# Order of the feed-forward products and of the Fourier steps changed, and U's remainders at a change of batch formed on Pool instead of VectorE

## The reference, cut to what matters

```python
# q, k, v: (2, 8, 768, 64); x below is (2, 768, 512); FF = 2048
x = local_and_global_attention(q, k, v)          # 96 local keys, 8 global ones
h = x.transpose(0, 2, 1) @ U @ V                 # rank 32, mixes the sequence
u = x + h.transpose(0, 2, 1)
x = u + relu(u @ w_ch1) @ w_ch2                  # layer 1, per batch
mixed = real(fft(fft(x, axis=1), axis=2))
u = x + mixed
un = (u - mean(u)) / sqrt(var(u) + 1e-6)
out = u + relu(un @ moe2_w_ch1) @ moe2_w_ch2     # layer 2, per batch
```

## Time and profile before

| what | value |
|---|---|
| median of 3 runs | 742.73 us (742.34 to 746.5) |
| profiled execution: its own time | 743.1 us |
| profiled execution: span of the core | 741.3 us |
| TensorE busy, share of the span | 682.5 us, 92% |
| VectorE / ScalarE / Pool busy | 421.2 / 308.4 / 377.6 us |

### The profile page before, as it was taken

How to read it: one execution, slowest core, us unless ns; L and a number is a source line. 1 busy time by engine, 2 the same in 40 slices (tenths; PEclk the granted TensorE clock), 3 DMA queues, 4 the chain that set the end, 5 groups by cost and what they waited for, 6 DMA issues and landing times.

```text
span 741.3 us, 10239 instructions
## 1 busy us (share of the span) xinstructions
PE 682.5 (92%) x3672; PEld 605.1 (82%) x3672; DVE 421.2 (57%) x903; ACT 308.4 (42%) x665; POOL 377.6 (51%) x365
## 2 busy tenths in 40 slices
PE   8949989999999988799997979999897889999997
PEld 6949889888898877688886869787786778899886
DVE  7526665544445386764675466653865485454544
ACT  4636676442433353234332444332343364334430
POOL 0140143244355899553453796555444876665621
PEclk9988999999999989999999999999999999999999
DMA  8332224012112313111110111111111022121132
GB/s 240 132 124 97 98 97 143 15 55 79 38 56 81 108 58 93 57 43 43 58 57 29 58 57 57 57 57 57 31 56 56 30 70 73 62 81 57 57 114 86
DMA packets 50532, 54.07 MB, mean 73 GB/s; under 512 B 4432, under 2 KB 37328, under 8 KB 50352
## 3 DMA queue, kind: packets, MB, share of 16 engines
q1 hardware_dynamic: 50480, 53.40, 22.9%
HBM read 53.39 MB, written 3.15 MB: 76 GB/s over the span
## 4 chain that ended last, share of the span: by engine, by line
PE 67%; DVE 12%; POOL 8%; ACT 6%; issue 5%; DMA 1%; DVEq 0%; SPq 0%; POOLq 0%; ACTq 0%
PE yP L753 10%; PE yP L755 9%; PE yP L754 9%; PE Yb L732 3%; PE Yb L733 3%; PE Yb L734 3%; PE aP L647 3%; PE aP L621 3%; PE Zb L732 2%; PE Zb L734 2%; PE Zb L733 2%; DVE Y L1249 2%; PE Xb L732 2%; PE Xb L733 2%; PE Xb L734 2%
## 5 line engine op out<-in xcount | busy, mean ns | idle before, releaser
L518 POOL TENSOR_TENSOR WCL<-w_stage,WCH 128x512 fp32r<-128x512 f32 (+1 forms) x128 | 154.7, 1230 | 204.9 <-ACT WCH L952 204.9
L1249 DVE TENSOR_TENSOR Y<-yP,Y 128x512 f32<-128x512 f32 x192 | 129.7, 684 | 89.4 <-PE yP L755 89.1
L753 PE MATMUL yP<-WOH,hidH 128*128 128x512 f32 x384 | 155.6, 405 | 24.6 <-DVE Y L1249 22.8
L755 PE MATMUL yP<-WOH,hidL 128*128 128x512 f32 x384 | 153.1, 399 | 0.0
L754 PE MATMUL yP<-WOL,hidH 128*128 128x512 f32 x384 | 152.6, 397 | 0.0
L524 POOL TENSOR_TENSOR WOL<-o_stage,WOH 128x512 fp32r<-128x512 f32 x64 | 86.0, 1366 | 46.6 <-ACT WOH L959 46.6
L753 PEld LDWEIGHTS yP<-WOH,hidH 128*128 128x128 f32 x384 | 73.5, 191 | 43.7 <-DVE Y L1249 28.2
L962 ACT ACTIVATE hidH<-Xb 128x384 fp32r<-128x384 f32 x64 | 31.4, 491 | 182.1 <-PE yP L755 174.3
L1242 DVE SCALAR_TENSOR_TENSOR hidL<-Xb,hidH 128x384 fp32r<-128x384 f32 x64 | 35.6, 556 | 89.8 <-ACT hidH L962 89.8
L755 PEld LDWEIGHTS yP<-WOH,hidL 128*128 128x128 f32 x384 | 73.0, 190 | 16.2
L754 PEld LDWEIGHTS yP<-WOL,hidH 128*128 128x128 f32 x384 | 73.3, 191 | 11.0
(11 more groups left out here) (216 smaller groups left out, 1360.3 us busy)
## 6 DMA issues: line engine op xcount, KB each, us to landing
w_stage<-w_in SPq DMA_DIRECT2D x128, 128.0 KB, 2.3
o_stage<-w_out SPq DMA_DIRECT2D x32, 512.0 KB, 3.3
V<-v_win SPq DMA_DIRECT2D x8, 704.0 KB, 7.0
K<-k_win SPq DMA_DIRECT2D x8, 644.0 KB, 5.4
Q<-q_t SPq DMA_DIRECT2D x16, 192.0 KB, 3.4
Y<-x_scratch SPq DMA_DIRECT2D x8, 384.0 KB
out<-Y SPq DMA_DIRECT2D x12, 256.0 KB, 3.7
CSraw<-seq_dft SPq DMA_DIRECT2D x1, 1348.0 KB, 7.3
```

Source lines behind the costliest of these rows:

```text
L518: nc.gpsimd.tensor_tensor(WCL[:, g % 2, u0:u1, :, :], w_stage[:, 1 + u0:1 + u1, :, :], hi32(WCH[:, g % 2, u0:u1, :, :]), ALU.subtract).the ...
L753: nc.tensor.matmul(bank[:, :], hh, WOH[:, h % 2, f, :], start=f == 0, stop=False)
L755: mm = nc.tensor.matmul(bank[:, :], hl, WOH[:, h % 2, f, :], start=False, stop=f == 1)
L1249: nc.vector.tensor_tensor(y, yP[t % 2][:, :], y, ALU.add).then_inc(s_yadd, 1)
```

## The change

- `ITEMS` becomes P1 P6 L0 P5 L1 P2 L2 L3 P7 L4 L5 P4 P3: P5 and P6 change places, and P3 and P4. The relu and `lo` of (f 1, half 1) move from P7 (ScalarE) and L4 (VectorE) to L5. The first output tiles wait for three of the round's four remainders, and only L3 for all four.
- `FFN_SLOT` is 35; the last `first_split` is at slot 33.
- The Fourier steps stand only in gaps 1 to 8 of a round (`CALM`), one position per gap, and `combine` is cut into `combine` and `stats`.
- ScalarE's UCH of a sum waits for that sum alone, of a RAW slice for none, and stands in other gaps.
- UCL at a change is formed by Pool in two instructions per factor, in its own order: four factors ahead of the change's round, P7's before `w_lo`, P4's and P3's behind it.
- Pool does `u_sums` ahead of `w_sums(g+2)`, and `u_sums(0, k)` ahead of `w_sums(1)`.
- CSH is made in three instructions, CSL in six, CDL in two.

```diff
-ITEMS = ("P1", "P5", "L0", "P6", "L1", "P2", "L2", "L3", "P7", "L4", "L5", "P3", "P4")
+ITEMS = ("P1", "P6", "L0", "P5", "L1", "P2", "L2", "L3", "P7", "L4", "L5", "P4", "P3")
+CALM = (1, 2, 3, 4, 5, 6, 7, 8)
...
-        FFN_SLOT = 33
+        FFN_SLOT = 35
...
-            for product, late in zip(PRODUCTS, (2, 4, 6, 7, 10, 13, 15)):
+            for product, late in zip(PRODUCTS, (3, 5, 7, 8, GAPS + 2, GAPS + 4, GAPS + 6)):
                 put(GAPS * (g - 1) + late, "split", c, product)
...
+            def at(n, *what):
+                put(GAPS * (first + n // len(CALM)) + CALM[n % len(CALM)], "fourier", b, *what)
+            for n, *what in ((0, "fold", 0, 0), (1, "fold", 0, 1), (2, "fold", 0, 2), (3, "split", 0), (4, "edge"), (6, "seq", 0, 0),
+                             (7, "fold", 1, 0), (8, "seq", 0, 1), (8, "fold", 1, 1), (9, "fold", 1, 2), (10, "split", 1),
+                             (12, "seq", 1, 0), (13, "seq", 1, 1), (15, "seq", 2, 0), (16, "mid")):
+                at(n, *what)
+            for n in range(18, 42):
+                for i in range(HT):
+                    for late, *what in ((0, "dim", i, 0), (1, "dim", i, 1), (2, "combine", i, 0), (3, "stats", i, 0), (4, "combine", i, 1),
+                                        (5, "stats", i, 1), (6, "norm", i, 0), (7, "norm", i, 1), (7, "turn", i, 0), (8, "turn", i, 1)):
+                        if n == 18 + 7 * i + late:
+                            at(n, *what)
...
+            def split(c, name):
+                j, op = PRODUCTS.index(name), FACTORS[name][1]
+                pool.wait_ge(s_uch, splits(c) + j + 1)
+                for k in range(KF):
+                    nc.gpsimd.tensor_tensor(UCL[:, op, k, :], factor(op)[:, k, :], hi32(UCH[:, op, k, :]), ALU.subtract).then_inc(s_ucl, 1)
             w_sums(0)
             w_lo(0)
-            w_sums(1)
             for k in range(KD):
                 u_sums(0, k)
+            w_sums(1)
             for g in range(ROUNDS):
+                if g in CHANGES:
+                    split(CHANGES.index(g), PRODUCTS[4])
                 if g + 1 < ROUNDS:
                     w_lo(g + 1)
+                if g in CHANGES:
+                    for name in PRODUCTS[5:]:
+                        split(CHANGES.index(g), name)
                 o_lo(g)
-                if g + 2 < ROUNDS:
-                    w_sums(g + 2)
+                if g + 1 in CHANGES:
+                    for name in PRODUCTS[:4]:
+                        split(CHANGES.index(g + 1), name)
                 if g + 2 in CHANGES:
                     for k in range(KD):
                         u_sums(CHANGES.index(g + 2) + 1, k)
+                if g + 2 < ROUNDS:
+                    w_sums(g + 2)
                 if g == FPAIRS - 1:
...
-                if j == 0:
-                    act.wait_ge(s_tadd, 2 * KD * (c + 2))
+                if op >= T1:
+                    act.wait_ge(s_tadd, 2 * KD * (c + 1) + {T1: 2, T2: 6, T4: 7, T3: 8}[op])
...
-                if t == 0:
-                    pe.wait_ge(s_hidl, 4 * (h + 1))
+                if t % HT == 0:
+                    pe.wait_ge(s_hidl, 4 * h + (3 if t == 0 else 4))
```

More of the change, by code:

```diff
@@ L373, in fourier_slots @@
         def fourier_slots(b):
[L374 to L390, removed]
+            first = FPAIRS * (b + 1) + 1
+            def at(n, *what):
[10 more added lines that the diff above has]
+                            at(n, *what)
         for b in range(B):
@@ L566, in _ @@
                     nc.gpsimd.tensor_copy(FIX[:, :], CSraw[:, HT * (CN + HALF):SEQ_COLS]).then_inc(s_csh, 1)
-                    nc.gpsimd.tensor_copy(CSH[:, :, :], CSdft).then_inc(s_csh, 1)
-                    pool.wait_ge(s_csh, 2)
-                    nc.gpsimd.tensor_tensor(CSL[:, :, :], CSdft, hi32(CSH[:, :, :]), ALU.subtract).then_inc(s_csplit, 1)
+                    for t in range(HT):
+                        nc.gpsimd.tensor_copy(CSH[:, t, :], CSdft[:, t, :]).then_inc(s_csh, 1)
+                    pool.wait_ge(s_csh, 1 + HT)
+                    for t in range(HT):
+                        for c in (slice(0, CN), slice(CN, CN + HALF)):
+                            nc.gpsimd.tensor_tensor(CSL[:, t, c], CSdft[:, t, c], hi32(CSH[:, t, c]), ALU.subtract).then_inc(s_csplit, 1)
                 if g == FPAIRS:
@@ L573, in _ @@
                     nc.gpsimd.tensor_copy(CDH[:, :, :], CDraw).then_inc(s_csh, 1)
-                    pool.wait_ge(s_csh, 4)
-                    nc.gpsimd.tensor_tensor(CDL[:, :, :], CDraw, hi32(CDH[:, :, :]), ALU.subtract).then_inc(s_csplit, 1)
+                    pool.wait_ge(s_csh, HT + 3)
+                    for k in range(KF):
+                        nc.gpsimd.tensor_tensor(CDL[:, k, :], CDraw[:, k, :], hi32(CDH[:, k, :]), ALU.subtract).then_inc(s_csplit, 1)
         @block.tensor
@@ L983, in item_done @@
                     relu(0, 0, Xb)
-                elif item == "P7":
+                elif item == "L5":
                     act.wait_ge(s_x22, g + 1)
@@ L1357, in fourier @@
                     nc.vector.tensor_tensor(y[:, DS + 1:D], y[:, DS + 1:D], right[:, DS - 1:0:-1], ALU.add).then_inc(s_u2, 1)
+                elif what == "stats":
+                    i, part = at
+                    n = HT * b + i
+                    y = Y[:, base + HT * part + i, :]
                     dve.wait_ge(s_u2, 2 * (2 * n + part) + 2)
@@ L1382, in fill @@
                         mix(*what)
-                    elif kind == "split":
-                        split(*what)
                     elif kind == "fourier":
```

38 lines of the change are left out of this document (20 added, 18 removed).

## The result

The change made the kernel slower. The median went from 742.81 us (five runs) to 765.81 us (five runs, 764.39 to 770.62), a ratio of 1.0307 with a 95% interval of 1.0275 to 1.0339. The forecast was 728.2 us, with a range of 717 to 739. The profiled execution took 770.62 us, its span is 768.6; it is the slowest of the five, 4.8 us above their median.

A forecast was written before the change was run, and what follows sets the result against it. The prediction took TensorE as the bound, so its waits count. Terms -8.9 + 4.5 + 1.6 - 6.2 - 4.5 - 1.0 = -14.5 took the profiled 743.1 us to 728.6, 728.2 as a median, range 717 to 739.

The forecast's parts named there:

- Part 1: Start, near 50 us: u_sums(0, k) ahead of w_sums(1) shrinks TensorE's 9.48 us wait to 2.4, without slow clock; -8.9 us.
- Part 2: Changes of batch: Pool forms U's remainders, its queue delaying P7, P4 and P3; +4.5 us at the first, +1.6 later.
- Part 3: Rounds 10 to 14 and 18 to 22: Fourier steps in the calm gaps remove TensorE's waits; -6.2 and -4.5 us.
- (b): Rival: Pool becomes the bound and runs slower than its rows, its stretches half longer; 796 us, chance 0.06.
- Part 4: Last round: L0 waits for the third remainder, not the fourth, while P3 runs; -1.0 us.
- (a): Rival: only the start gains; the calm gaps trade waits for others, so part 3's terms are 0; 738.9 us, chance 0.15.
- (c): Rival: later pairs' loads or a clock still at 0.5 hold the start, leaving 3 of 8.9 us; 734.1 us, chance 0.10.

The follow-up runs named there:

- e4: The kernel before, with only u_sums(0, k) put ahead of w_sums(1) on Pool: 735.88 us, ratio 0.9902.
- c1: The changed kernel with the Fourier steps back in the old gaps and U's remainders back on VectorE: 720.49 us, ratio 0.9682 against the kernel before.
- e1: The changed kernel with only its Fourier steps put back into the old gaps, over all 13: 735.39 us, ratio 0.9896 against the kernel before.
- e7: The changed kernel with Pool forming only a small part of W's remainders in rounds 9 to 13 and 17 to 21, the rest left out: 744.34 us.
- e5: The changed kernel with its own order of Fourier steps spread over all 13 gaps, 1.6 items apart: 738.53 us, ratio 0.9908 against the kernel before.
- e6: The changed kernel, calm gaps kept, with the turns and the second block's seq steps one gap later: 748.84 us, ratio 1.0066 against the kernel before.
- c2: c1 with all Fourier steps of batch 0 four gaps later: 722.08 us, ratio 0.9703 against the kernel before.
- c3: c1 with only the Fourier steps of the first eight slots of batch 0 four gaps later: 718.70 us, ratio 0.9657 against the kernel before.
- e3: The changed kernel with U's remainders at a change formed by VectorE again: 749.66 us, ratio 1.0098 against the kernel before.
- e9: e1 with the tables CSH and CSL formed behind o_lo(8), one round later: 742.61 us, ratio 0.998 against the kernel before.

## Why the prediction was wrong

**Part 1, the start: the wait right, the clock wrong, the total near partly by luck.** The wait is 2.38 us for 2.4 forecast, the first sum starts at 45.55 for 45.5, and P1(7) came 9.5 us earlier for 8.9. But I took the clock as not falling, on the word of rounds 15 and 16, where a wait of 2.65 us passed at full speed. Behind the same wait in round 7 the clock stood at 0.50 until 268.2:

```profile
262.00:268.00 6.00, 5.93 (x16) 5.07 (x17) 4.93 (x8) 4.40 (x6) 5.04 (x3) 0.50 0.31 87
```

The 0.84 of round 7 in the earlier trace rows was that warning. In the changed kernel the clock was at 0.50 from 50.0 to 53.4 us, a loss of 1.7 us where 1.8 were to be won, and e4 shows 0.74 in the window. By itself the step gave P1(0) 6.3 us (e4), less than my lower end of 7.0. In the changed kernel P1(0) starts only 2.2 us earlier (94.80 for 96.97) and the rest is won by P1(7): rounds 0 to 6 take 146.6 us for 153.9, 4.7 of it in round 2 alone. I had put all that at nothing. The later `FFN_SLOT` leaves fewer attention slots to their gaps and more ahead of them, so the two shifts belong together; that the sum of them is worth the 3 us beyond e4's 6.3 was not tried apart.

**Part 2, Pool at a change: right against the kernel before, and the wrong comparison.** P7's remainder was to end 36.7 us after P1(7) and ended 36.1 after; P7 was to wait 9.0 and waited 8.37; rounds 7 and 8 were to lose 4.3 more and lost 3.6, rounds 16 and 24 0.8 and lost 1.2. I counted 4.5 + 1.6 us for it. But part of what it replaced was VectorE's remainders held up by "all eight sums", and the change removes that hold as well. With both kernels in the new order, Pool's remainders cost 14.9 us (c1 against e1). Per factor VectorE took 0.9 to 2.1 us, and Pool 2.0 in a queue that was full already: busy 28.45 of 28.61 us in round 8. The Trainium skill's advice in "GPSIMD Engine Reference", section 4.1, which I named as speaking against this part, holds here in the measured 14.9 us.

Round 9 was to pay 0.2 and paid 2.9. The tables ended 8.1 us behind P1(9), as my queue had it (305.3 - 297.2 there, 295.10 - 286.99 in the trace), where they ended 3.7 behind it before (296.55 - 292.88). That later end alone does not make the 2.9: with a lighter Pool (e7) the tables end 8.1 us behind P1(9) as well, and the round takes 22.96 us, less than before the change. What differs is the first fold on VectorE. Its first four sums (EO and MIR) take 0.56, 0.55, 0.54 and 0.55 us in e7, and 1.60, 1.07, 1.00 and 1.62 beside Pool's remainders of W in the changed kernel.

**Part 3, the calm gaps: this step failed,** the terms -6.2 and -4.5, with -10.7 us forecast and +28.6 measured in the profiled execution; taking the gaps back won 30.4 us by the medians (e1). "Does the work fit the eight gaps?" was answered with an average: VectorE has 9.7 us to do in 13.6. It does fit; VectorE is busy 67.71 of 120.37 us in rounds 10 to 14. But TensorE does not wait for VectorE's average. It waits for the next link of a chain, and the eight gaps put the links one item apart (1.04 or 1.39 us), where before norm stood five items behind combine, and the turn five behind norm. A `combine` of two adds takes 0.84 us alone and up to 2.8 beside Pool; stats, root and norm another 2.3 (0.68 + 0.18 + 0.52 + 0.20 + 0.15 + 0.55), and a tile's add comes between. Of the wait of 4.78 us, 1.95 are what Pool added to the two adds. e5 (1.6 items apart: -27.3 us), e6 (one gap more before the turns: -17.0) and e7 (Pool out of the way: -21.5) show both halves of this. The price then about doubled through the clock, for which I had put nothing. I had both warnings in hand, the 5.32 us of the earlier trace rows and my own remark in rival (b) that combines have two SBUF inputs as well, and used them only for Pool's speed, not VectorE's.

The waits that I wanted gone by this, 6 us in each batch, went down to 4.0 us in e1 without any calm gap. The relu at L5 and the exchange of P5 and P6, which e1 keeps, are what could do it; they were not tried apart.

**Part 4, the end: right,** -1.1 for -1.0.

**The rivals.** (a) named the mechanism ("a fold or a combine now always stands ahead of a tile's add") and priced it at nothing lost. It should have carried a loss: its waits are new ones, not those of before under another name. (b), the rival on the slower side, was about Pool's rows growing; they did not (Pool's subtractions of 384 elements for U took 1.01 us in the mean, and P7's remainder ended on time), and the slower side, to which I gave 0.05, arrived by another way. (c) had the clock near 50 us at 0.50 "all the same"; that came, hidden in the total by the shorter rounds 0 to 6.

## What to carry to other kernels

In queues in program order, the price of a step's place is the distance to whoever needs its result, counted in the bound engine's work, against the chain's own length with contention in it. A load that fits on average says nothing about it: list the chain link by link, and give each link the time of the slowest row of its form. And where a change removes an old hold and moves work at the same time, compare the move also with the hold gone, or its price hides in the other's gain. Where two engines hold each other up, look at the length of the single instruction: what an add pays is the rest of the one that is running, so the long instructions are the ones to cut.

## What the runs showed of the hardware

TensorE's clock fell behind short waits. Windows of after, right behind the waits of 2.27 us (324.95), 2.15 (372.29) and round the one of 4.78 (410.88):

```profile
326.60:333.30 6.70, 6.70 (x19) 5.35 (x18) 1.69 (x4) 0.92 (x3) 0.68 (x1) 0.50 0.00 0
374.40:377.60 3.20, 3.20 (x14) 3.10 (x13) 0.00 (x0) 1.03 (x3) 0.00 (x0) 0.50 0.57 154
408.50:415.20 6.70, 4.32 (x12) 3.56 (x13) 3.75 (x9) 0.79 (x2) 1.78 (x3) 0.50 0.23 76
```

Stretches of 3.4 to 6.8 us at 0.50 (1.2 GHz; the windows above lie inside them) cost up to half their length, about as much as the waits themselves. The sum of the waits does not decide. e6, whose longest wait in these rounds is 2.1 us, keeps 1.00 in rounds 10 to 14 with 9.06 us of idle time; c2 has only 2.9 us of idle time there, nearly all of it in the one wait below, and the clock stood at 0.50 from 355.9 to 362.7:

```profile
356.51 0.80 PE L764 MATMUL yP<-WOH,hidH 128*128 128x512 f32 x1 [2.88 <-DVE Y L1264]
```

The length of a wait does not decide alone either. In the kernel before, the same wait of 2.65 us stands in rounds 7, 15 and 23 (up to 262.07, 433.13 and 593.29), and only the first was followed by a slow clock. The wait of 2.4 us near 47 us was followed by 6.8 us of it in e4 and e6, by 3.4 in after, and by none in c3, e3 and e9. What tells these apart the runs do not say.

VectorE's adds of two SBUF operands took 0.42 us alone and up to 1.5 beside one of Pool's instructions, which they waited out, and freeing Pool in the Fourier rounds was worth 21.5 us although Pool never held TensorE there. Cutting Pool's tables into small instructions changed who pays: VectorE's 5.32 us became 2.1 at most, and Pool's 5.76 became 7.35.
